# Experts in native float32 from an 8-slot weight ring, the MLP's matrices split on ACT and DVE in 16 pieces

## What is computed

```python
x = attention(q, k, v)                  # (2304, 512): 8 heads, 4 local, 4 strided
do_compute = x @ w_skip > 0
e_idx = argmax(x @ w_gate)              # one of 8 experts for a token
h = max(x[mask] @ w1[e], 0)             # w1[e]: 512 x 1024
y[mask] = gate_w[mask] * (h @ w2[e])    # w2[e]: 1024 x 512
x[do_compute] += y
h = x @ w_in                            # 512 x 2048
out = max(0.01 * h, h) @ w_out          # 2048 x 512
```

## Time and profile before

| | |
|---|---|
| time, median of 3 runs | 816.52 us (816.3 to 817.72) |
| span of the profiled execution | 812.8 us |
| time outside the span, from the two lines above | 3.7 us |
| PE busy | 725.0 us (89%) |
| DVE busy | 416.4 us (51%) |
| ACT busy | 346.3 us (43%) |
| POOL busy | 125.9 us (15%) |
| DMA | 91.09 MB, mean 112 GB/s |

### The profile page before, as it was taken

The page is one execution under the profiler, slowest core; times in us unless marked ns, Lnnn a source line. Parts: engine busy times, 40 slices in busy tenths (PEclk is TensorE's granted clock), DMA queues, the critical chain, the costliest instruction groups (busy, mean ns, idle before and its releaser), DMA issues.

```text
span 812.8 us, 13496 instructions
## 1 busy us (share of the span) xinstructions
PE 725.0 (89%) x4627; PEld 669.0 (82%) x4627; DVE 416.4 (51%) x781; ACT 346.3 (43%) x669; POOL 125.9 (15%) x114
## 2 busy tenths in 40 slices
PE   3989989963687799996699999999999999999997
PEld 2888889853687799995599998999999999999996
DVE  4766748664888888886332234223333332333222
ACT  4688776431454477775122232222322222223222
POOL 2120134024624511110300100100100010000000
PEclk9999979895898899998699999999999999999999
DMA  8584664793566678886300120120011012001001
GB/s 176 120 180 104 157 173 120 244 358 112 198 220 218 199 232 266 253 259 226 116 1 1 40 78 0 40 79 1 10 50 58 0 39 77 0 0 40 1 0 40
DMA packets 75165, 91.09 MB, mean 112 GB/s; under 512 B 25809, under 2 KB 46801, under 8 KB 75122
## 3 DMA queue, kind: packets, MB, share of 16 engines
q1 hardware_dynamic: 70386, 78.66, 32.8%
q0 software_dynamic: 3680, 11.86, 4.7%
q10 hardware_dynamic: 1056, 0.02, 0.1%
HBM read 73.88 MB, written 16.65 MB: 111 GB/s over the span
## 4 chain that ended last, share of the span: by engine, by line
PE 73%; SPq 9%; DVE 6%; issue 5%; DMA 4%; ACT 3%; POOL 0%; ACTq 0%; DVEq 0%; POOLq 0%
PE psum L1605 25%; PE psum L1622 24%; PE psum L1531 6%; SPq L415 5%; PE psum L1517 5%; PE psum L1533 2%; SPq L410 2%; DVE hp L1225 2%; PE psum L1519 2%; DMA x_rows<-xo 2%; PE psum L1455 1%; PE psum L1472 1%; SPq L400 1%; PE psum L1542 1%; PE psum L1357 1%
## 5 line engine op out<-in xcount | busy, mean ns | idle before, releaser
L1295 DVE SCALAR_TENSOR_TENSOR g_act<-g_raw 128x384 f32<-128x384 f32 x96 | 53.7, 559 | 221.1 <-ACT g_raw L964 220.6
L964 ACT ACTIVATE g_raw<-psum 128x384 f32<-128x384 f32 x96 | 47.2, 492 | 236.8 <-PE psum L1605 236.8
L1605 PE MATMUL psum<-x2h,wih 128*128 128x384 f32 x384 | 131.6, 343 | 1.4 <-DVE x2l L1277 1.4
L1605 PE MATMUL psum<-x2h,wil 128*128 128x384 f32 x384 | 130.2, 339 | 0.0
L1605 PE MATMUL psum<-x2l,wih 128*128 128x384 f32 x384 | 129.7, 338 | 0.0
L1622 PE MATMUL psum<-wh,g_l 128*128 128x512 f32 x288 | 114.0, 396 | 0.0
L1622 PE MATMUL psum<-wl,g_h 128*128 128x512 f32 x288 | 113.7, 395 | 0.0
L1622 PE MATMUL psum<-wh,g_h 128*128 128x512 f32 x288 | 112.2, 389 | 0.5 <-DVE g_l L1299 0.5
L1186 DVE TENSOR_TENSOR wl<-raw,wh 128x1024 fp32r<-128x1024 f32 x67 | 90.9, 1359 | 13.6 <-ACT wh L861 13.2
L1531 PE MATMUL psum<-hp,wh 128*128 128x320 f32 x256 | 78.6, 376 | 20.9 <-DVE hp L1225 20.7
L1299 DVE TENSOR_TENSOR g_l<-g_act,g_h 128x384 fp32r<-128x384 f32 x96 | 53.7, 559 | 57.0 <-ACT g_h L971 57.0
(11 more groups left out here) (163 smaller groups left out, 1177.7 us busy)
## 6 DMA issues: line engine op xcount, KB each, us to landing
raw<-in_moe_w_dram SPq DMA_DIRECT2D x64, 512.0 KB, 4.0
q_st<-in_q_dram SPq DMA_DIRECT2D x8, 576.0 KB
k_st<-in_k_dram SPq DMA_DIRECT2D x8, 576.0 KB
x<-x_rows SPq DMA_DIRECT2D x6, 768.0 KB, 5.4
y_rows<-zrow SPq DMA_DIRECT2D x1, 4480.0 KB
x_sb<-x_rows SPq DMA_DIRECT2D x4, 1024.0 KB, 6.2
wi_raw<-in_moe_w_in_dram POOLq DMA_DIRECT2D x4, 1024.0 KB, 5.8
raw<-in_moe_w_out_dram SPq DMA_DIRECT2D x8, 512.0 KB, 3.8
```

The costliest lines, as they stand in the source:

```text
L964: act.activation(g_raw[:, f % 2, :], bank[f % 2][:, 0:MT * P], ACT.Copy).then_inc(s_mr, 1)
L1295: dve.scalar_tensor_tensor(out=g_act[:, f % 2, :], in0=g_raw[:, f % 2, :], scalar=LEAK, in1=g_raw[:, f % 2, :], op0=ALU.mult, op1=ALU.max) ...
L1605: last = pe.matmul(bank[f % 2][:, 0:MT * P], wt[:, c, f * P:(f + 1) * P], xp[:, T.par, c, :], start=(c == 0 and n == 0), stop=(c == KD - 1 ...
```

## The change

Expert matmuls read float32 operands directly. `wring` has eight slots, one for each piece of an expert, and PE reads the weights where SP puts them; nothing splits them, nor x, nor the hidden units. ACT applies the relu straight out of PSUM, and ACT and DVE each copy a half of the gathered x and of the tile's output. SP refills a slot when PE has used it (`half_done`), in the order 0, 2, 1, 4, 3, 6, 5, 7. SP also waits once for the zero fill of the y rows before tile 0. POOL no longer splits anything: it loads w_in and w_out in eight loads of 1 MB into a two-slot stage, one a tile. In each of the eight tiles ACT casts two pieces (after chunks 2 and 6) and DVE subtracts them. The MLP reads `woh` and `wol` for w_out. ACT and DVE have the eight tiles written out, where they had a loop. The MLP's program is otherwise the same, with some buffers at other addresses.

```diff
         def half_load(eng, e_, n):
-            u_, to = n // 2, raw[:, n % 4, :]
+            u_, to = n // 2, wring[:, n, :]
...
-            eng.dma_start(to, src).then_inc(s_raw[n % 4], 16)
+            eng.dma_start(to, src).then_inc(s_w[n], 16)
...
+        def stage_piece(n):
+            i, r_ = n // 2, n % 2
+            src = stage[:, i % 2, 1024 * r_:1024 * r_ + 1024]
+            if i < NU:
+                f0 = i * (F2 // NU)
+                view = (slice(None), slice(2 * r_, 2 * r_ + 2), slice(f0, f0 + F2 // NU))
+                return wih[view], wil[view], src.rearrange("p (c f) -> p c f", f=F2 // NU)
+            view = (slice(None), i - NU, slice(1024 * r_, 1024 * r_ + 1024))
+            return woh[view], wol[view], src
...
# SP, a tile
-                def slot_free(n):
-                    k_ = i0 * 2 * NU + ((d + 1) * 2 * NU + n - 3)
-                    sp.wait_ge(s_wh, k_)
-                    sp.wait_ge(s_wl, k_)
+                def half_done(n):
+                    k_ = i0 * FC + (d * FC + 2 * (n // 2) + 2)
+                    sp.wait_ge(s_l2 if n % 2 else s_l1, k_)
...
-                    for n in range(2 * NU):
-                        y_before(n)
-                        slot_free(n)
+                    for n in (0, 2, 1, 4, 3, 6, 5, 7):
+                        if n == 1:
+                            y_before()
+                        half_done(n)
                         half_load(sp, ex_, n)
...
+            sp.wait_ge(s_zd, 32)
             tile(0, 0)
...
# POOL
-            for n in range(5):
-                pool.wait_ge(s_raw[n % 4], 16 * (n // 4 + 1))
-                split(half(wh, n), half(wl, n), raw[:, n % 4, :], s_wh, s_wl, n + 1)
...
-                pool.wait_ge(s_wi, 16 * (i + 1))
-                w_ = slice(i * (F2 // NU), (i + 1) * (F2 // NU))
-                split(wih[:, :, w_], wil[:, :, w_],
-                      wi_raw[:, :].rearrange("p (c f) -> p c f", f=F2 // NU), s_wih, s_wil, i + 1)
-                pool.wait_ge(s_wil, i + 1)
...
+            stage_load(0)
+            for i in range(2 * NU):
                 pool.wait_ge(s_xt, 2 * (i + 1))
                 gather_x(i + 1)
+                if i + 1 < 2 * NU:
+                    if i:
+                        pool.wait_ge(s_stl, 2 * i)
+                    stage_load(i + 1)
...
# ACT, a tile
-                    act.activation(hb[:, f % 2, :], bank[f % 2][:, TILE:2 * TILE], ACT.Copy
-                                   ).then_inc(s_hb, 1)
+                    act.activation(hp[:, f % 4, :], bank[f % 2][:, 0:TILE], ACT.Relu
+                                   ).then_inc(s_hp, 1)
...
+                    if base and f in (2, 6):
+                        n = 2 * T.d + f // 4
+                        act.wait_ge(s_st[T.d % 2], 16 * (T.d // 2 + 1))
+                        hi, _, src = stage_piece(n)
+                        act.activation(hi, src, ACT.Copy).then_inc(s_sth, 1)
...
+                act.activation(yt[:, 0:2, :], Y[:, 0:2, 0:TILE], ACT.Copy).then_inc(s_ya, 1)
...
# DVE, a tile
+                if not first:
+                    y_rows(T.i0 + (T.d - 1))
+                def stage_lo(n):
+                    dve.wait_ge(s_sth, n + 1)
+                    hi, lo, src = stage_piece(n)
+                    dve.tensor_tensor(lo, src, hi.bitcast(F32), ALU.subtract).then_inc(s_stl, 1)
+
+                if base:
+                    stage_lo(2 * T.d)
+                x_copy(T.i0 + (T.d + 1), 1 - par)
+                if base:
+                    stage_lo(2 * T.d + 1)
+                dve.wait_ge(s_l2, T.n(FC, FC))
...
+                dve.tensor_copy(yt[:, 2:4, :], Y[:, 2:4, 0:TILE]).then_inc(s_yv, 1)
...
# PE
             def hidden(T, f):
...
-                pe.wait_ge(s_wl, T.n(8, 2 * u_ + 1))
+                if r_ == 0:
+                    pe.wait_ge(s_w[2 * u_], T.n(16, 16))
                 if not (T.first and f < 2):
-                    pe.wait_ge(s_ht, T.n(FC, f - 1))
+                    pe.wait_ge(s_hp, T.n(FC, f - 1))
...
-                    pe.matmul(bank[f % 2][:, 0:2 * TILE], wh[:, u_, w_], xt[:, T.par, c, :],
-                              start=(c == 0), stop=False)
-                    last = pe.matmul(bank[f % 2][:, 0:TILE], wl[:, u_, w_], xt[:, T.par, c, 0:TILE],
-                                     start=False, stop=(c == KD - 1))
+                    last = pe.matmul(bank[f % 2][:, 0:TILE], wring[:, 2 * u_, w_], xt[:, T.par, c, :],
+                                     start=(c == 0), stop=(c == KD - 1))
```

More of the change, by code:

```diff
@@ L267, in attention_experts_mlp @@
         s_plan = sem("s_plan")
[L269 to L274, removed]
+        s_w = [sem(f"s_w{i}") for i in range(2 * NU)]
+        s_st = [sem("s_st0"), sem("s_st1")]
+        s_sth = sem("s_sth")
+        s_stl = sem("s_stl")
         s_tick = sem("s_tick")
@@ L886, in tile @@
                     act.wait_ge(s_l1, T.n(FC, f + 1))
[L887 to L890 removed]
+                    if not (first and f < 4):
+                        act.wait_ge(s_l2, T.n(FC, f - 3))
+                    act.activation(hp[:, f % 4, :], bank[f % 2][:, 0:TILE], ACT.Relu
+                                   ).then_inc(s_hp, 1)
@@ L907, in relu @@
-                    def relu(f=f):
-                        act.wait_ge(s_ht, T.n(FC, f + 1))
-                        if not (first and f < 4):
-                            act.wait_ge(s_l2, T.n(FC, f - 3))
-                        act.activation(hp[:, f % 4, 0:TILE], ht[:, f % 2, :], ACT.Relu
-                                       ).then_inc(s_hh, 1)
-                    for stage in ((weights, relu) if f < FC - 1 else (relu, weights)):
-                        stage()
-                act.wait_ge(s_l2, T.n(FC, FC))
@@ L917, in tile @@
-                for c in (0, 2):
-                    act.activation(yb[:, c:c + 2, :], Y[:, c:c + 2, TILE:2 * TILE], ACT.Copy
-                                   ).then_inc(s_ya, 1)
-            tile(Tile(0, 0))
-            with act.Fori(0, E // 2 - 1) as i2:
-                for u in range(2):
-                    tile(Tile(i2 * 2, u + 1))
-            tile(Tile(0, E - 1))
+                    if base and f in (2, 6):
[3 more added lines that the diff above has]
+                        act.activation(hi, src, ACT.Copy).then_inc(s_sth, 1)
@@ L926, in _ @@
+                act.wait_ge(s_l2, T.n(FC, FC))
+                if not first:
+                    act.wait_ge(s_yt, T.n(2, 0))
+                act.activation(yt[:, 0:2, :], Y[:, 0:2, 0:TILE], ACT.Copy).then_inc(s_ya, 1)
+            for d in range(E):
+                tile(Tile(0, d), base=True)
             with act.If(tiles > E):
@@ L940, in _ @@
             y_rows(last_tile)
-            for n in (5, 6, 7):
-                half_hi(n, tiles * 32 + 32)
             def x2_hi(m, j, par):
@@ L966, in mstep @@
                     act.wait_ge(s_mg, T.n(FC2, f + 1))
-                    if T.first and f == 0:
-                        act.wait_ge(s_wl, tiles * 8 + 8)
                     if not (T.first and f < 2):
@@ L1238, in _ @@
-            tile(Tile(0, 0))
-            with dve.Fori(0, E // 2 - 1) as i2:
-                for u in range(2):
-                    tile(Tile(i2 * 2, u + 1))
-            tile(Tile(0, E - 1))
+                if not first:
+                    y_rows(T.i0 + (T.d - 1))
[3 more added lines that the diff above has]
+                    dve.tensor_tensor(lo, src, hi.bitcast(F32), ALU.subtract).then_inc(s_stl, 1)
@@ L1243, in _ @@
+                if base:
+                    stage_lo(2 * T.d)
+                x_copy(T.i0 + (T.d + 1), 1 - par)
+                if base:
+                    stage_lo(2 * T.d + 1)
+                dve.wait_ge(s_l2, T.n(FC, FC))
+                if not first:
+                    dve.wait_ge(s_yt, T.n(2, 0))
+                dve.tensor_copy(yt[:, 2:4, :], Y[:, 2:4, 0:TILE]).then_inc(s_yv, 1)
+            for d in range(E):
+                tile(Tile(0, d), base=True)
             with dve.If(tiles > E):
@@ L1257, in _ @@
             y_rows(last_tile)
-            for n in (5, 6, 7):
-                half_lo(n, tiles * 8 + n + 1)
             def x2_rows(m):
```

177 lines of the change are left out of this document (59 added, 118 removed).

## The result

The changed kernel takes 785.29 us (median of 4 runs, 784.71 to 785.62); the kernel before, on the same chip, 816.41 us (4 runs, 813.73 to 817.72). The ratio is 0.9631, with a 95% interval of 0.9608 to 0.9653. The sign was forecast, the size was not: 793.7 us was predicted, and 785.29 lies 3.7 us under the low end of the range.

What follows compares the result with a forecast made beforehand. Late expert tiles were taken as bound by PE, early ones by DVE held up beside POOL. Stalls removed, less dearer matmuls, gain 22.8 us: span 812.8 to 790.0, plus 3.7 outside, gives 793.7 us; range 789 to 803.

Steps and rivals of the forecast that it cites:

- The stalls of tiles 0 to 3 go: Early expert tiles: PE's waits for DVE, held up beside POOL's split of w_in, vanish; some 30 us.
- A native half of 0.136 us: Expert matmuls: each half of a float32 matmul on 160 columns takes 0.136 us, from attention's 0.85 ns a column.
- The rival that counts columns alone: Expert matmuls: 0.267 us native against 0.200 a pair, so PE loses 34 us instead of 7; 821 us, chance 0.02.
- A pair of 0.258 us: Late expert tile: a split pair takes 0.258 us, so native matmuls add 0.9 us and a tile lasts 19.2.
- The start, 0.5 us counted: Start of expert stage: first matmul at 198.5 instead of 198.99, as ACT and DVE copy halves of x together.
- That wait stays as it is: Before the last y_turn: PE's 4.34 us wait, marked "issue", is unchanged, so nothing is gained there.
- Time outside the span: Whole kernel: the median stands 3.7 us above the profiled span.
- DMA at 313 GB/s in full: Expert tiles: full DMA rate estimated at 313 GB/s, so a tile's 5.9 MB take 18.8 of 19.2 us.
- the casts: Rival, expert tiles: casts in ACT's order hold up relus, up to 17 us, 811 us at worst; chance 0.03.
- the stall that stays: Rival, early tiles: w_in's traffic, not POOL's instructions, makes them slow, so stalls remain; 824 us, chance 0.02.
- the slow halves: Rival, expert matmuls: a half costs 0.18 us like a pair's first matmul, 49 us lost; 843 us, chance 0.04.
- the DMA's pace: Rival, expert tiles: DMA stays at 269 GB/s and PE waits on pieces in tiles 5 to 7; 800 us, chance 0.12.

Runs made afterwards that it cites:

- experiment 1: Kernel before, only w_in's split taken from POOL: ACT casts and DVE subtracts it in 16 pieces over the eight tiles; fp32r pairs stay. 789.05 us, ratio 0.9673.
- Experiments 2 and 3: Kernel before with SP holding tile 1's first weight loads until tile 0's x_turn: 813.45 us; the same plus w_in split by ACT and DVE, not POOL: 785.9 us.
- experiment 5: Changed kernel with added DRAM-to-DRAM copies behind each stage load: one of 1 MB, 785.48 us, ratio 0.9639; two, 804.36 us, ratio 0.986.
- experiment 2: Kernel before, SP waiting for tile 0's x_turn before it loads tile 1's first weights: 813.45 us, ratio 0.9977 (0.9951 to 1.0004).
- experiment 4: Changed kernel with the splits of w_in and w_out given back to POOL in all eight tiles, none on ACT and DVE: 783.55 us, ratio 0.962.

## Why the prediction came out as it did

- **The stalls of tiles 0 to 3 go, some 30 us: right**, in mechanism and size. All seven tiles after the first are alike, and experiment 1 shows the cause.
- **A native half of 0.136 us: right**, measured 0.136. The rival that counts columns alone was right on the native matmul (0.267 us, measured 0.272) and wrong on the pair (0.200, measured 0.263), and so promised 34 us lost on PE; the rows decided rightly.
- **A pair of 0.258 us: too little.** The step divided a stretch of 18.0 us by the work of a tile of 18.28. A pair is 0.263 us, a tile pays 0.6 us for native matmuls instead of 0.9 and lasts 18.86 instead of 19.2. This is 2.7 us over eight tiles, by arithmetic that the rows before allowed.
- **The start, 0.5 us counted, 3.0 measured: the step that failed most.** "ACT and DVE now copy halves of x" was seen; what stood ahead of it, the gather with SP's first load beside it, was not. The prediction had SP's new order of loads before it, and judged it only for the refills of the ring. Experiments 2 and 3 show the 2.1 us of the load; the other 0.9 us are the shorter copy (0.5) and a router that ended 0.5 us earlier in this profile. The latter is chance: in the ten profiles without the load the first hidden matmul comes between 194.61 and 197.38.
- **"That wait stays as it is": wrong**, by 2.0 us up to the MLP. The branch starts when the sequencer is free of its last wait, whatever the matmuls still have to do, and the change moved that wait forward. It lasts 3.73 to 5.25 us in the nine profiles that have it, so a part of such a difference is chance. The sequencer's records would have told it; the row "issue" alone did not.
- **Time outside the span: 3.7 us taken, 1.8 measured** (784.71 less 782.9, the profiled execution). Every other run shows 1.7 to 2.3. The median of before had been set against the span of an execution that was itself some 2 us faster: its stalls vary from run to run. Against the median after, 2.4 us lie outside, so this is 1.3 us of the miss.
- **DMA at 313 GB/s in full: wrong**, without effect on the time. The forecast counted on slack; there was capacity too (experiment 5).
- **The clock**: half speed until 201.1 from a start at 195.96, 2.6 us lost where 2.4 were counted. Right.
- **Prices of two rivals**: a half of 0.18 us instead of 0.136 would cost 45 us and not 49, so 839 us, and a quarter of the casts' 17 us gives 798 and not 797. Neither bears on the outcome.

The miss of 8.4 us is thus, but for rounding, 2.5 at the start, 2.3 in the tiles, 2.0 behind them, 0.2 in the MLP and 1.3 outside the span. All five lie on one side, partly by chance (the router, the branch's length), and the range had no room for terms that are small one by one: its low end of 789 gave 4.7 us to the halves and the clock alone. Of the rivals, the stall that stays, the slow halves, the columns and the casts each fell by the rows above; the DMA's pace fell by experiment 5.

## What to carry to other kernels

A slow instruction may be the work of a neighbouring engine: where a small instruction lasts as long as another engine's large one beside it, move the large one or take the small one out of the chain, before rewriting the arithmetic. When a change moves a load, look at every latency-bound transfer that it stood beside, and when it makes a result come sooner, ask which delay that work does not shorten (a branch) stood behind that result. A gain at one place is worth nothing while a later bound can swallow it (experiment 2), so test parts together as well as alone.

## What was not expected of the hardware

- A taken branch of PE over the code for further tiles holds it for 3.7 to 5.3 us (5.25 before, 4.82 after, 4.73 when run again, 3.73 in experiment 4); it costs what is left of it when the last share ends.
- One load of 512 KB issued 0.3 us behind a gather made that gather 4.80 to 5.16 us long (three profiles) instead of 2.88 to 3.15 (ten).
- A DVE instruction with both inputs in SBUF is held beside POOL's cast (2.01 us instead of 0.32) as beside its subtraction (4.61); DVE copies out of PSUM, 0.49 us, are not.
- The DMA moves 374 GB/s over a tile, 362 over the stage, without a wait on PE; at 368 with two copies queued, a single piece took 19.46 us.
- A wait of 4.0 us on PE in a full tile is dear: the clock falls to half behind it (230 to 234), so tiles of 18.86 became 24.8.
